# Attention with pooled queries and a two-layer network: the small scores and the ninth block at the end of a step, the row maximum in two parts

## The chip, the cores and the metric

The kernel runs on one core of a Trainium2 chip. The metric is the time of one execution on the device in microseconds (us); the time before is the median of three runs. Profiles come from one further execution, recorded by the hardware profiler.

## The reference

There are 4 batches of 8 heads, 1152 keys and a head size of 64. Two neighbouring queries are averaged, so each head has 576 queries. The output of attention, with the heads side by side, goes through two matrix products with a leaky activation between them.

```python
q_pool = q.reshape(B, H, S // 2, 2, D).mean(axis=3)
scores = scale * np.matmul(q_pool, k.transpose(0, 1, 3, 2))
scores = scores - np.max(scores, axis=-1, keepdims=True)
attn = np.exp(scores)
attn = attn / (np.sum(attn, axis=-1, keepdims=True) + 1e-09)
attn_out = np.matmul(attn, v)
x = attn_out.transpose(0, 2, 1, 3).reshape(B * S, H * D)
h = x @ w_in
g = np.maximum(h, 0.0) + alpha * np.minimum(h, 0.0)
out = g @ w_out
```

## The kernel before

**Steps.** The heads are worked in 16 pairs. The 1152 queries of a pair are nine tiles of 128; tile 4 takes 64 queries of each head. A step `s` handles one tile against all 1152 keys, so attention has 144 steps, `s % 9` is the step's place t in a round of nine, and "step 4" below means a step with t = 4. Each engine has its own instruction stream, and the order in it is written out by hand in `step` functions; engines meet by semaphores only. Odd and even steps use two buffers of scores in PSUM (`S_AT`) and two halves of `e_sb`.

**What TensorE does in step s (L575 to L604).** It waits for `exp_done`, the large exponential of tile s, and for the two slots. Then it transposes the first eight blocks of 128 columns of the tile's exponentials in 16 matmuls, one half of the 128 rows into slot 0 and the other into slot 1 (L584). It waits for `ninth_free` and for `exp_cut_done`, the small exponential of tile s + 1. Then come the small scores of tile s + 2, 128 columns (L517), the transpose of the ninth block of tile s into `NINTH` (L544), the big scores of tile s + 2, 1024 columns (L529), and a part of the product of exponentials and values (`product`, L570). `PRODUCT` says which: steps 5 to 8 work on group 0 (tiles 0 to 4 of this pair, 320 columns for each head), steps 0 to 4 on group 1 of the pair before (tiles 5 to 8, 256 columns). Nearly all take two of the nine key blocks; step 8 takes three and step 4 one. Steps 6 and 1 first spread the inverted sums of a group over the partitions (L554, into slot 0). In steps 7 and 8, `begin_scores` also waits for the keys and queries of the next pair.

**PSUM.** The small scores of both buffers and `NINTH` lie in different columns of the same bank, the third of `s_ps`. The big scores have two banks in each buffer, each slot has one, and the product has one.

**What VectorE does (L455 to L472).** It copies slot 1 to `pt` (L464) and frees the slot, copies the ninth block (L466) and frees it, and takes the negated row maximum of tile s + 2 over all 1152 columns (L431) as soon as all its scores are there (`s_ready`, 2). In steps 4 and 8 it inverts the sums of a group before that (L449, L453), in step 5 it casts x (L445). `scale` multiplies a finished product by the inverted sums (L439); it stands at the start of steps 0 and 5.

**What ScalarE does (L352 to L370).** It waits for `max_ready` of tile s + 1, takes the exponential of the 128 small columns with `accum_out` (L341), copies slot 0 to `pt` (L357), and takes the exponential of the 1024 large columns (L348). After the spreads it copies them to `inv_bc` (L363) and frees slot 0.

GpSimd sums the pairs of queries and takes the low part of x; SyncE issues the loads, of which those of values wait for `v_free`, which VectorE raises in step 5. The network behind attention is not touched, except that VectorE's first scaling there moves into the last step.

Of the kernel before, what the change touches and what calls it, by code (L numbers as in the profile page):

```python
# [7 lines left out]
ALU = mybir.AluOpType  # L8
# [3 lines left out]
P = 128  # L12
BANK = 512


def build(nc, q, k, v, w_in, w_out, alpha, out):
# [41 lines left out]
    with ExitStack() as ctx:  # L58
# [19 lines left out]
        neg_max = sb("neg_max", [P, 2])  # L78
        row_sum = sb("row_sum", [P, 2, TILES])
# [29 lines left out]
        NINTH = s_ps[:, 2 * BANK + P:2 * BANK + 2 * P]  # L109
# [20 lines left out]
        s_ready = sem("s_ready")  # L130
        max_ready = sem("max_ready")
# [3 lines left out]
        ninth_ready = sem("ninth_ready")  # L135
        slot_free = [sem(f"slot{i}_free") for i in range(2)]
        ninth_free = sem("ninth_free")
# [289 lines left out]
        def _(dve):  # L427
            def row_max(s):
                b = s % 2
                dve.wait_ge(s_ready, 2).then_inc(s_ready, -2)  # L430
                nc.vector.tensor_reduce(out=neg_max[:, b:b + 1], in_=s_ps[:, S_AT[b]:S_AT[b] + NKEY],  # L431
                                        op=ALU.max, axis=AX_X, negate=True).then_inc(max_ready, 1)
# [22 lines left out]
            def step(s, pair, left=2):  # L455
                t, g = s % TILES, s // TILES % 2
                if t == 0 and pair is not None:
                    dve.wait_ge(x_sb_free, 1).then_inc(x_sb_free, -1)
                    scale(0)
                if t == 5 and pair is not None:  # L460
                    scale(1)
                    dve.sem_inc(v_free[1 - g], 1)
                dve.wait_ge(tr_ready[1], 1).then_inc(tr_ready[1], -1)  # L463
                nc.vector.tensor_copy(pt_half(t, 1), half_columns(slot_ps[1][:, :])).then_inc(slot_free[1], 1)  # L464
                dve.wait_ge(ninth_ready, 1).then_inc(ninth_ready, -1)
                nc.vector.tensor_copy(pt_ninth(t), ninth_columns(t)).then_inc(ninth_free, 1)  # L466
# [4 lines left out]
                if left > 1:  # L471
                    row_max(s + 2)  # L472
# [20 lines left out]
            dve.sem_inc(ninth_free, 1)  # L493
            dve.sem_inc(pv_free, 1)
            row_max(0)
            row_max(1)
            over_steps(dve, step)
            dve.wait_ge(alpha_in, 16).then_inc(alpha_in, -16)
            dve.wait_ge(x_sb_free, 1).then_inc(x_sb_free, -1)
            scale(0)  # L500
# [11 lines left out]
        def _(pe):  # L512
# [62 lines left out]
            def step(s, pair, left=2):  # L575
# [12 lines left out]

                pe.wait_ge(ninth_free, 1).then_inc(ninth_free, -1)
                if left > 0:  # L590
                    pe.wait_ge(exp_cut_done, 1).then_inc(exp_cut_done, -1)  # L591
                if left > 1:
                    begin_scores(s + 2)
                    small_scores(s + 2)
                transposed(s, 2 * CH, NINTH).then_inc(ninth_ready, 1)
                if left > 1:
# [104 lines left out]
```

## Time and profile before

| | us |
|---|---|
| Median of three runs | 1018.21 (1015.3 to 1018.55) |
| The profiled execution | 1016.51 |
| Its span, first to last instruction | 1014.0 |
| Start, up to the transposes of step 8 | 58.67 |
| Steps 8 to 142 | 537.70 |
| The last step and the network | 417.63 |
| TensorE busy (matmuls) | 919.4 (91%) |
| VectorE busy | 528.3 (52%) |
| ScalarE busy | 423.4 (42%) |

Engines are called PE (TensorE matmul), PEld (TensorE weight load), DVE (VectorE), ACT (ScalarE), POOL (GpSimd) and SP (SyncE). A row of a timeline gives the start, the time that the merged instructions span, the engine and line, the output and inputs, their number, and in brackets the idle time before with what ended it. "PEq L591" is the semaphore wait in line 591. The ends of matmuls are modelled, so two groups can overlap by some hundredths; where one group follows another, the distance of the starts is the safer measure. The granted clock of TensorE is given as a share of 2.4 GHz.

### The profile page before, as it was taken

Reading aid. Unit: us, or ns where it says so; the run is one execution under the profiler, and the core shown is the slowest. Engines: PE = TensorE matmul, PEld = TensorE weight load, DVE = VectorE, ACT = ScalarE, POOL = GpSimd, SP = SyncE. Lnnn points to the kernel's source line nnn. Section 1 sums busy time; section 2 is a strip of 40 time slices with the busy share of each in tenths; the row PEclk is TensorE's granted clock in tenths of the full one; section 3 lists DMA queues with packets and bytes.
Section 4 is the critical chain, followed back from the end, with each engine's and each line's share of the span. In section 5 each row is a group of like instructions: output and inputs, shape, how many; then the busy total and the mean of one; then the engine's idle time right before and its main releaser. Section 6 shows DMA issues by size and latency. Waiting matters only on the chain. (4 is left out here: it accounts for less than half of the span.)

```text
span 1014.0 us, 20768 instructions
## 1 busy us (share of the span) xinstructions
PE 919.4 (91%) x6896; PEld 632.5 (62%) x6896; DVE 528.3 (52%) x836; ACT 423.4 (42%) x963; POOL 213.6 (21%) x182
## 2 busy tenths in 40 slices
PE   3798888889889888888888889999999999999997
PEld 1344444444444444444444459999999999999996
DVE  1456666666666666666666644444444444444442
ACT  1455555555555555555555542222232222322222
POOL 2011112102111111211111023333333333333331
PEclk9899999999999999999999999999999999999999
DMA  7334134224423413532442012122232222422211
GB/s 171 97 77 123 49 75 122 64 57 122 104 63 76 122 47 75 122 87 60 96 121 65 1 32 63 62 62 63 62 125 62 62 63 62 126 63 67 60 48 62
DMA packets 36366, 79.57 MB, mean 78 GB/s; under 512 B 5360, under 2 KB 9456, under 8 KB 36336
## 3 DMA queue, kind: packets, MB, share of 16 engines
q1 hardware_dynamic: 33936, 74.48, 28.4%
q10 hardware_dynamic: 2400, 4.72, 1.3%
q8 instruction: 16, 0.26, 0.1%
q14 instruction: 14, 0.11, 0.0%
HBM read 74.46 MB, written 4.72 MB: 78 GB/s over the span
## 5 line engine op out<-in xcount | busy, mean ns | idle before, releaser
L431 DVE TENSOR_REDUCE neg_max<-s_ps 128x1 f32<-128x1152 f32 x144 | 195.5, 1357 | 111.3 <-DVEq L430 111.3
L529 PE MATMUL s_ps<-k_f,q_f 64*128 64x512 f32 (+1 forms) x640 | 167.6, 657 | 5.2 <-PEq L540 5.2
L570 PE MATMUL pv_ps<-pt,v_f 128*64 128x256 f32 (+1 forms) x1152 | 170.3, 417 | 0.0
L348 ACT ACTIVATE e_sb<-s_ps,neg_max 128x1024 f32<-128x1024 f32 x144 | 160.3, 1113 | 0.0
L341 ACT ACTIVATE e_sb<-s_ps,neg_max 128x128 f32<-128x128 f32 x144 | 53.0, 368 | 221.2 <-ACTq L340 221.1
L570 PEld LDWEIGHTS pv_ps<-pt,v_f 128*64 128x64 f32 x1152 | 71.4, 137 | 112.5 <-issue 82.8
L464 DVE COPY pt<-slot_ps 128x512 f32<-128x512 f32 x144 | 99.5, 691 | 75.6 <-DVEq L463 75.5
L517 PE MATMUL s_ps<-k_end,q_f 128*128 128x128 f32 (+1 forms) x320 | 68.1, 317 | 77.6 <-PEq L591 56.4
L584 PEld LDWEIGHTS slot_ps<-ident,e_sb 64*128 64x128 f32 x2304 | 86.1, 141 | 71.1 <-issue 71.1
L613 PE MATMUL slot_ps<-x_hi,wi_hi 128*128 128x384 f32 x384 | 129.5, 337 | 1.0 <-PEq L609 1.0
L613 PE MATMUL slot_ps<-x_lo,wi_hi 128*128 128x384 f32 x384 | 129.5, 337 | 0.0
L613 PE MATMUL slot_ps<-x_hi,wi_lo 128*128 128x384 f32 x384 | 129.0, 336 | 0.0
L477 DVE TENSOR_SCALAR e_sb<-slot_ps,alpha_sb 128x384 f32<-128x384 f32 x96 | 59.3, 618 | 123.7 <-DVEq L475 123.7
L584 PE MATMUL slot_ps<-ident,e_sb 64*128 64x64 f32 x2304 | 104.6, 231 | 4.0 <-PEq L579 3.8
L486 DVE TENSOR_TENSOR g_lo<-e_sb,g_hi 128x384 fp32r<-128x384 f32 x96 | 53.6, 559 | 99.2 <-DVEq L485 99.2
L517 PEld LDWEIGHTS s_ps<-k_end,q_f 128*128 128x128 f32 (+1 forms) x320 | 42.6, 182 | 93.4 <-issue 91.4
L628 PE MATMUL s_ps<-wo_lo,g_hi 128*128 128x512 f32 x240 | 95.1, 396 | 0.0
L628 PE MATMUL s_ps<-wo_hi,g_lo 128*128 128x512 f32 x240 | 94.8, 395 | 0.0
L628 PE MATMUL s_ps<-wo_hi,g_hi 128*128 128x512 f32 x240 | 93.3, 389 | 1.1 <-PEq L625 1.1
L272 POOL TENSOR_TENSOR q_raw<-q_raw 128x576 f32<-128x576 f32 x32 | 44.9, 1404 | 234.4 <-POOLq L271 234.4
L357 ACT ACTIVATE pt<-slot_ps 128x512 f32<-128x512 f32 x144 | 85.1, 591 | 19.5 <-ACTq L356 19.5
L303 POOL TENSOR_TENSOR wo_lo<-wo_raw,wo_hi 128x512 fp32r<-128x512 f32 x48 | 62.0, 1292 | 139.1 <-POOLq L302 139.1
(46 smaller groups left out, 1006.3 us busy)
## 6 DMA issues: line engine op xcount, KB each, us to landing
q_raw<-in_q SPq DMA_DIRECT2D x64, 288.0 KB, 4.6
k_f<-in_k SPq DMA_DIRECT2D x64, 288.0 KB, 4.1
wi_raw<-in_w_in SPq DMA_DIRECT2D x48, 256.0 KB, 2.6
wo_raw<-in_w_out SPq DMA_DIRECT2D x48, 256.0 KB, 2.6
v_f<-in_v SPq DMA_DIRECT2D x32, 288.0 KB, 3.1
out<-pt ACTq DMA_DIRECT2D x6, 768.0 KB, 4.6
k_end<-in_k SPq DMA_DIRECT2D x64, 32.0 KB, 4.0
alpha_sb<-in_alpha SPq DMA_DIRECT2D x1, 8.0 KB, 4.7
```

Of the source, the lines that this page charges most:

```text
L303: nc.gpsimd.tensor_tensor(wo_lo[i][:, :], wo_raw[i][:, :], wo_hi[i][:, :].bitcast(F32), ALU.subtract).then_inc(pool_self, 1)
L348: nc.scalar.activation(e_sb[:, b * NKEY + at:b * NKEY + at + n], s_ps[:, S_AT[b] + at:S_AT[b] + at + n], ACT.Exp, bias=neg_max[:, b:b + 1] ...
L357: nc.scalar.activation(pt_half(t, 0), half_columns(slot_ps[0][:, :]), ACT.Copy).then_inc(slot_free[0], 1)
L431: nc.vector.tensor_reduce(out=neg_max[:, b:b + 1], in_=s_ps[:, S_AT[b]:S_AT[b] + NKEY], op=ALU.max, axis=AX_X, negate=True).then_inc(max_r ...
L464: nc.vector.tensor_copy(pt_half(t, 1), half_columns(slot_ps[1][:, :])).then_inc(slot_free[1], 1)
L477: nc.vector.tensor_scalar(neg_sb, hid, 0.0, alpha_sb[:, bass.ds(f, 1)], ALU.min, ALU.mult).then_inc(dve_self, 1)
L517: ins = nc.tensor.matmul(s_ps[to:to + m, S_AT[b] + at:S_AT[b] + at + P], q_f[2 * g + h][:, first:first + m], k_end[2 * g + h][:, end, :], ...
L529: ins = nc.tensor.matmul(s_ps[to:to + m, S_AT[b] + at:S_AT[b] + at + BANK], q_f[2 * g + h][rows, first:first + m], k_f[2 * g + h][rows, at ...
L570: ins = nc.tensor.matmul(pv_ps[h * D:(h + 1) * D, 0:n], v_f[2 * g + h][:, a, :], pt[:, a, at:at + n], start=(a == 0), stop=(a == KT - 1))
L584: ins = nc.tensor.transpose(slot_ps[i][:, a * HALF:(a + 1) * HALF], e_sb[rows, at:at + P], ident[rows, rows])
L613: ins = nc.tensor.matmul(slot_ps[h][:, 0:TOK], w[i][:, d * P:(d + 1) * P], x[:, at:at + TOK], start=(d == 0 and w is wi_hi and x is x_hi), ...
L628: ins = nc.tensor.matmul(y_ps[h][t], g[h][:, t * P:(t + 1) * P], w[i][:, :], start=(first == 0 and j == 0), stop=(last == 1 and j == 2))
```

## The change

In TensorE's step, the big scores of tile s + 2 follow the transposes of tile s directly, then comes the product, and at the step's end the transpose of the ninth block, the wait for `exp_cut_done`, and the small scores of tile s + 2. `NINTH` now lies in the first 128 columns of slot 1; so the slot is taken and freed twice in a step, and `ninth_free` is gone. VectorE takes the maximum over the 1024 large columns (`big_max`) once the big scores are there, and the maximum over the 128 small columns with the minimum of the two negated values (`row_max`) at the start of the next step. The scalings move from the start of steps 0 and 5 to steps 8 and 4, ahead of the copy of the ninth block, which is now last in VectorE's step.

```diff
-        NINTH = s_ps[:, 2 * BANK + P:2 * BANK + 2 * P]
+        NINTH = slot_ps[1][:, 0:P]
...
-            def row_max(s):
+            def big_max(s):
                 b = s % 2
                 dve.wait_ge(s_ready, 2).then_inc(s_ready, -2)
-                nc.vector.tensor_reduce(out=neg_max[:, b:b + 1], in_=s_ps[:, S_AT[b]:S_AT[b] + NKEY],
-                                        op=ALU.max, axis=AX_X, negate=True).then_inc(max_ready, 1)
+                nc.vector.tensor_reduce(out=neg_big[:, b:b + 1],
+                                        in_=s_ps[:, S_AT[b] + BIG_AT[b]:S_AT[b] + BIG_AT[b] + 2 * BANK],
+                                        op=ALU.max, axis=AX_X, negate=True).then_inc(max_self, 1)
+            def row_max(s):
+                b = s % 2
+                dve.wait_ge(s_end_ready, 1).then_inc(s_end_ready, -1)
+                nc.vector.tensor_reduce(out=neg_end[:, b:b + 1],
+                                        in_=s_ps[:, S_AT[b] + END[b][0]:S_AT[b] + END[b][0] + P],
+                                        op=ALU.max, axis=AX_X, negate=True).then_inc(max_self, 1)
+                dve.wait_ge(max_self, 2).then_inc(max_self, -2)
+                nc.vector.tensor_tensor(neg_max[:, b:b + 1], neg_big[:, b:b + 1], neg_end[:, b:b + 1],
+                                        ALU.min).then_inc(max_ready, 1)
...
             def step(s, pair, left=2):
                 t, g = s % TILES, s // TILES % 2
-                if t == 0 and pair is not None:
-                    dve.wait_ge(x_sb_free, 1).then_inc(x_sb_free, -1)
-                    scale(0)
-                if t == 5 and pair is not None:
-                    scale(1)
-                    dve.sem_inc(v_free[1 - g], 1)
+                if left > 0:
+                    row_max(s + 1)
                 dve.wait_ge(tr_ready[1], 1).then_inc(tr_ready[1], -1)
                 nc.vector.tensor_copy(pt_half(t, 1), half_columns(slot_ps[1][:, :])).then_inc(slot_free[1], 1)
-                dve.wait_ge(ninth_ready, 1).then_inc(ninth_ready, -1)
-                nc.vector.tensor_copy(pt_ninth(t), ninth_columns(t)).then_inc(ninth_free, 1)
+                if left > 1:
+                    big_max(s + 2)
                 if t in INVERT:
                     invert(INVERT[t])
                 if t == 5 and pair is not None:
                     x_high(pair + (0 if s < 2 * TILES else 1))
-                if left > 1:
-                    row_max(s + 2)
+                if t == 4 and s >= TILES:
+                    scale(1)
+                    dve.sem_inc(v_free[1 - g], 1)
+                if t == 8:
+                    dve.wait_ge(x_sb_free, 1).then_inc(x_sb_free, -1)
+                    scale(0)
+                dve.wait_ge(ninth_ready, 1).then_inc(ninth_ready, -1)
+                nc.vector.tensor_copy(pt_ninth(t), ninth_columns(t)).then_inc(slot_free[1], 1)
...
-                pe.wait_ge(ninth_free, 1).then_inc(ninth_free, -1)
-                if left > 0:
-                    pe.wait_ge(exp_cut_done, 1).then_inc(exp_cut_done, -1)
                 if left > 1:
                     begin_scores(s + 2)
-                    small_scores(s + 2)
-                transposed(s, 2 * CH, NINTH).then_inc(ninth_ready, 1)
-                if left > 1:
                     for ins in big_scores(s + 2):
                         ins.then_inc(s_ready, 1)
                 group, tiles = PRODUCT[t]
...
                     product(group, g if group == 0 else 1 - g, tiles)
+                pe.wait_ge(slot_free[1], 1).then_inc(slot_free[1], -1)
+                transposed(s, 2 * CH, NINTH).then_inc(ninth_ready, 1)
+                if left > 0:
+                    pe.wait_ge(exp_cut_done, 1).then_inc(exp_cut_done, -1)
+                if left > 1:
+                    small_scores(s + 2).then_inc(s_end_ready, 1)
```

## Rows read from the trace of the kernel before

**Rows 1.** Stretches: the steady part of attention, steps 8 to 142.

```profile
core 0: us, PE busy (x) PEld busy (x) DVE busy (x) ACT busy (x) POOL busy (x), PEclk, DMA share, GB/s
58.67:596.37 537.70, 473.45 (x4572) 246.23 (x4571) 337.50 (x510) 293.05 (x705) 77.16 (x69) 1.00 0.33 81
```

**Rows 2.** The page's groups: busy us, mean ns, idle before, releaser.

```profile
L431 DVE TENSOR_REDUCE neg_max<-s_ps 128x1 f32<-128x1152 f32 x144 | 195.5, 1357 | 111.3 <-DVEq L430 111.3
L517 PE MATMUL s_ps<-k_end,q_f 128*128 128x128 f32 (+1 forms) x320 | 68.1, 317 | 77.6 <-PEq L591 56.4
```

**Rows 3.** Timeline of TensorE: start us, us; steps 6, 8, 0, 3, 4, 5.

```profile
412.07 0.77 PE L554 MATMUL slot_ps<-ident,inv_sum 128*64 128x128 f32 x12
412.67 1.25 PE L570 MATMUL pv_ps<-pt,v_f 128*64 128x320 f32 x8
413.91 0.71 PE L584 MATMUL slot_ps<-ident,e_sb 64*128 64x64 f32 x16
...
420.56 1.83 PE L570 MATMUL pv_ps<-pt,v_f 128*64 128x320 f32 x12
422.32 0.71 PE L584 MATMUL slot_ps<-ident,e_sb 64*128 64x64 f32 x16
422.96 0.49 PE L517 MATMUL s_ps<-k_end,q_f 128*128 128x128 f32 x2
...
436.34 1.08 PE L570 MATMUL pv_ps<-pt,v_f 128*64 128x256 f32 x8
437.35 0.71 PE L584 MATMUL slot_ps<-ident,e_sb 64*128 64x64 f32 x16
...
438.97 0.27 PE L544 MATMUL s_ps<-ident,e_sb 128*128 128x128 f32 x1
439.17 1.13 PE L529 MATMUL s_ps<-k_f,q_f 64*128 64x512 f32 x4
440.23 0.65 PE L570 MATMUL pv_ps<-pt,v_f 128*64 128x256 f32 x4
440.82 0.71 PE L584 MATMUL slot_ps<-ident,e_sb 64*128 64x64 f32 x16
442.57 0.46 PE L517 MATMUL s_ps<-k_end,q_f 128*128 128x128 f32 x2 [1.04 <-PEq L591]
...
443.07 1.13 PE L529 MATMUL s_ps<-k_f,q_f 64*128 64x512 f32 x4
```

**Rows 4.** Timeline of VectorE: the scalings, step 4, and step 5.

```profile
422.58 0.49 DVE L439 TENSOR_TENSOR x_sb<-pv_ps,inv_bc 128x320 f32<-128x320 f32 x1 [0.41 <-DVEq L438]
423.42 0.69 DVE L464 COPY pt<-slot_ps 128x512 f32<-128x512 f32 x1 [0.35 <-DVEq L463]
...
439.39 0.29 DVE L466 COPY pt<-s_ps 128x128 f32<-128x128 f32 x1 [0.45 <-DVEq L465]
439.60 0.16 DVE L449 SCALAR_TENSOR_TENSOR sum_eps<-row_sum 128x5 f32<-128x5 f32 x1
439.90 0.19 DVE L453 RECIPROCAL inv_sum<-sum_eps 128x5 f32<-128x5 f32 x1
440.49 1.36 DVE L431 TENSOR_REDUCE neg_max<-s_ps 128x1 f32<-128x1152 f32 x1 [0.39 <-DVEq L430]
441.76 0.41 DVE L439 TENSOR_TENSOR x_sb<-pv_ps,inv_bc 128x256 f32<-128x256 f32 x1
442.62 0.69 DVE L464 COPY pt<-slot_ps 128x512 f32<-128x512 f32 x1 [0.44 <-DVEq L463]
...
443.50 0.45 DVE L445 CAST x_hi<-x_sb 128x576 f32 x1
```

**Rows 5.** Timeline of ScalarE: the exponentials in step 5.

```profile
441.97 0.37 ACT L341 ACTIVATE e_sb<-s_ps,neg_max 128x128 f32<-128x128 f32 x1 [1.85 <-ACTq L340]
442.23 0.19 ACT L341 ACTIVATION_READ_ACCUMULATOR e_sb<-s_ps,neg_max 128x1 f32 x1
...
443.80 0.21 ACT L348 ACTIVATION_READ_ACCUMULATOR e_sb<-s_ps,neg_max 128x1 f32 x1
```

**Rows 6.** Stretches: two pieces of the first round, columns as in rows 1.

```profile
39.00:41.00 2.00, 1.04 (x18) 0.61 (x16) 1.49 (x2) 0.15 (x3) 0.00 (x0) 1.00 0.00 0
45.00:47.00 2.00, 1.52 (x5) 1.11 (x7) 0.80 (x2) 1.92 (x5) 0.00 (x0) 0.50 0.00 0
```

More of the change, by code:

```diff
@@ L78, in build @@
         neg_max = sb("neg_max", [P, 2])
+        neg_big = sb("neg_big", [P, 2])
+        neg_end = sb("neg_end", [P, 2])
         row_sum = sb("row_sum", [P, 2, TILES])
@@ L130, in build @@
         s_ready = sem("s_ready")
+        max_self = sem("max_self")
         max_ready = sem("max_ready")
@@ L135, in build @@
         ninth_ready = sem("ninth_ready")
+        s_end_ready = sem("s_end_ready")
         slot_free = [sem(f"slot{i}_free") for i in range(2)]
-        ninth_free = sem("ninth_free")
         inv_ready = sem("inv_ready")
@@ L427, in _ @@
         def _(dve):
+            def big_max(s):
+                b = s % 2
+                dve.wait_ge(s_ready, 2).then_inc(s_ready, -2)
+                nc.vector.tensor_reduce(out=neg_big[:, b:b + 1],
+                                        in_=s_ps[:, S_AT[b] + BIG_AT[b]:S_AT[b] + BIG_AT[b] + 2 * BANK],
+                                        op=ALU.max, axis=AX_X, negate=True).then_inc(max_self, 1)
             def row_max(s):
                 b = s % 2
-                dve.wait_ge(s_ready, 2).then_inc(s_ready, -2)
-                nc.vector.tensor_reduce(out=neg_max[:, b:b + 1], in_=s_ps[:, S_AT[b]:S_AT[b] + NKEY],
-                                        op=ALU.max, axis=AX_X, negate=True).then_inc(max_ready, 1)
+                dve.wait_ge(s_end_ready, 1).then_inc(s_end_ready, -1)
[5 more added lines that the diff above has]
+                                        ALU.min).then_inc(max_ready, 1)
             def scale(group):
@@ L492, in _ @@
                 dve.sem_inc(slot_free[i], 1)
-            dve.sem_inc(ninth_free, 1)
             dve.sem_inc(pv_free, 1)
+            big_max(0)
             row_max(0)
-            row_max(1)
+            big_max(1)
             over_steps(dve, step)
             dve.wait_ge(alpha_in, 16).then_inc(alpha_in, -16)
-            dve.wait_ge(x_sb_free, 1).then_inc(x_sb_free, -1)
-            scale(0)
             for n in range(PASSES):
@@ L637, in _ @@
             begin_scores(0)
-            small_scores(0)
+            small_scores(0).then_inc(s_end_ready, 1)
             for ins in big_scores(0):
@@ L641, in _ @@
             begin_scores(1)
-            big_scores(1)
+            for ins in big_scores(1):
+                ins.then_inc(s_ready, 1)
             pe.wait_ge(exp_cut_done, 1).then_inc(exp_cut_done, -1)
-            small_scores(1).then_inc(s_ready, 2)
+            small_scores(1).then_inc(s_end_ready, 1)
             over_steps(pe, step)
@@ L650, in _ @@
             pe.wait_ge(slot_free[1], 1)
-            pe.wait_ge(ninth_free, 1).then_inc(ninth_free, -1)
             product(1, 1, (0, 1))
```

## The prediction

> **What bounds the kernel now.** I first asked the stretches of the profile where the time lies. The steady part of attention runs from the transposes of step 8 to those of step 143, 135 steps, 537.70 us, or 35.85 us for each round of nine steps [rows 1]. The change touches only this part and the eight steps ahead of it, so nothing is expected to move in the feed-forward part. TensorE is busy in 473 of these 537.70 us. That share alone would suggest an engine near its limit, but the groups of instructions on the page show a hole: before the small scores TensorE stood idle for 77.6 us, 56.4 of it at L591, the wait for `exp_cut_done` [rows 2].
>
> Next I followed one hole through the timelines of three engines. The big scores of step 4 start at 439.17 [rows 3]. The row maximum starts at 440.49, 1.32 later, and takes 1.36, to 441.85 [rows 4]. The cut exponential starts 0.12 later, at 441.97, and its accumulator read ends at 442.42 [rows 5]. TensorE's small scores start 0.15 later, at 442.57, after 1.04 of idle time, and the next big scores at 443.07 [rows 3]. The loop is closed: 1.32 + 1.36 + 0.12 + 0.45 + 0.15 + 0.50 = 3.90 us for a step. Nine such steps are 35.1; the round has 0.75 more, since steps with a spread (0.60), with the third product tile or with new keys are longer on TensorE alone. So the kernel is bound by a ring through three engines, with the row maximum as its longest piece. TensorE has slack in most steps, and VectorE's other work (inversion, scaling, the cast of x) lies in VectorE's own holes, beside the ring.
>
> **What the change does to that ring.** The big scores no longer stand behind `exp_cut_done`. They follow the transposes at once. From transposes to the next matmul it takes 0.64 when nothing is late (422.32 to 422.96), from big scores to product 1.06 (439.17 to 440.23) [rows 3]. A product of two tiles takes 1.01 for 256 columns (436.34 to 437.35) and 1.24 for 320 (412.67 to 413.91), one tile 0.59 (440.23 to 440.82), three tiles 1.76 (420.56 to 422.32), all from start to the next group's start [rows 3]. The wait at L591 goes away: `exp_cut_done` is now asked for only at the step's end.
>
> **What it adds.** The reduction of 1152 columns is split. Copies of 512 and of 128 columns took 0.69 and 0.29 [rows 4], which is 1.04 ns for each column more; a reduction of 1024 columns is then, as an estimate, 1.36 - 128 x 1.04 ns = 1.23, and one of 128 about 0.29. The minimum of two columns has no row; the nearest is the 128x5 operation with 0.15 to 0.16, then 0.14 until the dependent one starts [rows 4]. Its bounds are 0.1 and 0.3. The end maximum, the minimum and their gap, 0.6 together, stand at the start of the next step while TensorE transposes (0.71), and VectorE could copy the half only when that is done. So I cost them at nothing there. If that cover went they would cost 0.6 in each step.
>
> The small maximum is also the head of the exponentials' chain: with the small scores ending about when the next transposes start, the minimum is out 0.64 after that start, the cut exponential starts at 0.76, and from the cut's start to the end of the large exponential's accumulator read are 2.04 (441.97 to 444.01) [rows 5], then 0.15 to TensorE: 2.95. Every step below is longer, so this chain waits for nobody.
>
> The ninth block is the piece that matters. Before, its copy was released to TensorE most of a step ahead of its use, as it had its own columns. Now it is put into slot 1, and the next step's transposes wait for `slot_free[1]`. If N is the start of the ninth transpose, its copy starts at N + 0.42 (438.97 to 439.39) and takes 0.29 [rows 3, 4]. From the copy's end to a matmul on TensorE there is no row; ScalarE to TensorE took 0.15, VectorE to ScalarE 0.12 [rows 3, 5]. I take 0.15. So the transposes start at N + 0.86, where TensorE alone, with 0.20 for the ninth block and 0.30 for the small scores out of the 0.50 above, would be ready at N + 0.50. This is a new wait of 0.36.
>
> And VectorE must reach that copy: in its queue stand, ahead of it, the large maximum, in steps 4 and 8 the inversion and a scaling, in step 5 the cast. The large maximum starts 0.64 + 1.32 = 1.96 after the transposes and ends at 3.19. A following instruction that is not late starts 0.08 before that end (439.60 against 439.39 + 0.29), so at 3.11. A scaling takes 0.84 to 0.86 until the next copy starts (422.58 to 423.42, 441.76 to 442.62), the inversion 0.30 and 0.19 [rows 4].
>
> **The sum, step by step**, each from its transposes to the next ones. Steps 0, 2 and 3: N = 0.64 + 1.06 + 1.01 = 2.71, copy at 3.13, next step at 3.57. Step 1: a spread of eight matmuls, 0.5 (between two thirds of the 0.60 that twelve took and all of it), gives 4.07. Step 4: inversion from 3.11 to 3.60, scaling from 3.52, copy at 4.38, next step at 4.82. Step 5: the cast (0.45) from 3.11, copy at 3.48, next step at 3.92. Step 6: 0.64 + 1.06 + 0.60 + 1.24 + 0.86 = 4.40. Step 7: 3.80. Step 8: the product starts at 1.70 and its last matmul ends 1.83 later, the scaling starts 0.19 after that end (422.58 against 422.39) at 3.72, copy at 4.56, next step at 5.00. The sum is 36.72 a round against 35.85: the bare steps win 0.33 each, and steps 4 and 8 give back more than all of it, because the scaling now stands between TensorE and its slot. Over 15 rounds that is +13.0. In the first eight steps there is no scaling, and about four bare steps win 0.33: -1.4. In all +11.6 us. The profiled execution took 1016.5 us (its span is 1014.0), the median is 1018.2; I set the forecast against the median: about 1029.
>
> The Trainium skill (VectorE: DVE Perf Modes, "Rules for kernel authors") advises to minimise the number of VectorE operations, which speaks against two instructions more in each step. By that rule alone, VectorE's time grows by about 0.32 a step, 46 us over 144 steps if VectorE were the bound; by the rows, it stood idle for 111.3 us before the row maxima alone [rows 2], and the sum charges nothing for the split itself.
>
> **Rivals.**
> *The hand-back is cheap (the other side).* If VectorE hands a slot to TensorE in less than 0.15, all nine steps shorten, as all end on that hand-over. The point from which it decides is 11.6 / 135 = 0.09 us less than taken, that is 0.06. At zero the sum is 11.6 - 20.3 = -8.7, 1009.5 us. Against it: both cross-engine hand-overs in the rows took 0.12 to 0.15. For it: no row shows this pair.
> *No change.* The gaps of 0.35 and 0.44 behind a scaling [rows 4] might not be paid in steps 4 and 8. Then a round is 0.8 shorter, the total -12, and the time 1018. Against it: the copy behind the scaling at 441.76 had its data already (those transposes, from 440.82, were over at 441.53) [rows 3, 4], so the gap belongs to the semaphore instructions behind the scaling, and these stay.
> *The clock falls.* In the first round, where a step had no product of the other group, TensorE was busy for 1.04 of 2.00 us, and shortly after ran at 0.50 of its clock, the 1.2 GHz level [rows 6]. Step 4 would now be busy for 2.8 of 4.82 us, with some 2.0 idle in one piece. If the clock fell there in every round, step 5's matmuls, 3.44 us at the full level, would need 6.9, which is 3.0 above the 3.92 of the sum: +45 us, 1074; in half of the rounds, 1051. Against it: before, step 5 bore 1.04 of idle time in one piece [rows 3] at a clock of 1.00 in the whole stretch [rows 1]. The Trainium skill (TensorE: Matmul & The Clock Gate, "What's actually happening") says that the throttled state is the default and activity releases it; by it this case is possible in a step so empty, and the trace agrees in the first round.
> *Waits laid bare.* Between the short small scores and the transposes TensorE now handles three waits. The gap of 0.44 behind a scaling had four semaphore instructions [rows 4], about 0.1 each. If 0.1 a step came on top it would be +13.5, 1043.
>
> **How the numbers follow.** The forecast as summed, with or without some bare waits, has 0.55; the clock 0.13; the cheap hand-back 0.18; no change 0.12; the rest is for what I have not seen. A difference of 0.3% is about what a measurement of this kernel tells from no change. The steps of the sum are built from rows that repeat to a hundredth, but an error of 0.1 in the common hand-over alone moves the total by 13.5, so the range goes from near the cheap hand-back, 1010, to half the clock case, 1051. Faster 0.18, same 0.13, slower 0.69.
>
> **What would show it.** Right: idle time before the transposes with the wait for the slot as releaser, some 0.36 in steps 1, 6 and 7 and over 1 in steps 4 and 8; no idle time before the big scores; bare steps of 3.57; a large maximum of 1.23; the minimum out before the half's copy. Wrong: bare steps near 3.4 would mean a cheap hand-back, matmuls of the big scores with twice their time the clock case, and a late large exponential before the transposes a chain that I take for hidden.

## The result, and the profile after

The changed kernel took 1049.1 us (median; 1046.19 to 1050.17), the kernel before 1017.7. The ratio is 1.0308, with a 95% interval of 1.0279 to 1.0337: slower, as forecast, but by 31 us where 11 were forecast, and inside the range (1010 to 1051) only by a hair. The profiled execution took 1050.17 us, with a span of 1047.3.

The page of the changed kernel, busy time by engine and three of its groups (busy us, mean ns, idle before and its releaser):

```profile
PE 910.0 (87%) x6896; PEld 631.0 (60%) x6896; DVE 584.1 (56%) x1124; ACT 418.5 (40%) x963; POOL 213.3 (20%) x182
...
L435 DVE TENSOR_REDUCE neg_big<-s_ps 128x1 f32<-128x1024 f32 x144 | 176.1, 1223 | 53.4 <-DVEq L434 52.9
L600 PE MATMUL slot_ps<-ident,e_sb 64*128 64x64 f32 x2304 | 105.2, 231 | 90.7 <-PEq L595 90.7
...
L545 PE MATMUL s_ps<-k_f,q_f 64*128 64x512 f32 (+1 forms) x640 | 168.5, 647 | 5.3 <-PEq L556 5.3
```

The wait for `exp_cut_done`, 56.4 us before [rows 2], is gone, and the big scores no longer wait for it. In its place stand 90.7 us of idle time ahead of the transposes, ended by L595, the wait for the slots. The large maximum takes 1223 ns, as estimated.

The stretches, with the granted clock behind the five busy times:

```profile
50.39:629.62 579.23, 471.41 (x4570) 248.02 (x4571) 390.30 (x779) 288.43 (x705) 77.10 (x69) 0.97 0.31 75
629.62:1047.00 417.38, 409.80 (x2089) 368.41 (x2089) 169.13 (x295) 110.53 (x212) 125.19 (x97) 1.00 0.23 70
0.00:50.39 50.39, 28.83 (x238) 14.57 (x239) 24.63 (x51) 19.59 (x46) 11.06 (x16) 1.00 0.59 141
```

The same cuts as before: up to the transposes of step 8 it took 50.39 us against 58.67, from there to the transposes of step 143 it took 579.23 against 537.70 [rows 1], and the rest is unchanged. So the first eight steps won 8.3 us and the 15 rounds lost 41.5. The granted clock in the rounds was 0.97, where it had been 1.00 [rows 1].

Now one hole, in steps 4 and 5 of a round. The timeline of TensorE, VectorE and the first ScalarE operation:

```profile
419.32 0.72 PE L600 MATMUL slot_ps<-ident,e_sb 64*128 64x64 f32 x16 [0.36 <-PEq L595]
...
419.84 1.11 PE L545 MATMUL s_ps<-k_f,q_f 64*128 64x512 f32 x4
...
421.10 1.22 DVE L435 TENSOR_REDUCE neg_big<-s_ps 128x1 f32<-128x1024 f32 x1 [0.23 <-DVEq L434]
421.46 0.33 PE L560 MATMUL slot_ps<-ident,e_sb 128*128 128x128 f32 x1
421.63 0.39 PE L533 MATMUL s_ps<-k_end,q_f 128*128 128x128 f32 x2
...
422.24 0.15 DVE L465 SCALAR_TENSOR_TENSOR sum_eps<-row_sum 128x5 f32<-128x5 f32 x1
422.54 0.19 DVE L469 RECIPROCAL inv_sum<-sum_eps 128x5 f32<-128x5 f32 x1
422.80 0.42 DVE L455 TENSOR_TENSOR x_sb<-pv_ps,inv_bc 128x256 f32<-128x256 f32 x1
423.67 0.29 DVE L490 COPY pt<-slot_ps 128x128 f32<-128x128 f32 x1 [0.44 <-DVEq L489]
...
424.11 0.71 PE L600 MATMUL slot_ps<-ident,e_sb 64*128 64x64 f32 x16 [2.09 <-PEq L595]
424.30 0.16 DVE L447 TENSOR_TENSOR neg_max<-neg_big,neg_end 128x1 f32<-128x1 f32 x1
424.58 0.37 ACT L344 ACTIVATE e_sb<-s_ps,neg_max 128x128 f32<-128x128 f32 x1 [2.68 <-ACTq L343]
```

The step is 4.79 us long (4.82 forecast). TensorE starts its last work at 421.63 and then stands idle for 2.09 us, while VectorE works through maximum, inversion, scaling and the copy of the ninth block. That copy ends at 423.96 and the transposes start at 424.11: the hand-over from VectorE to TensorE, for which no row stood before, takes 0.15. In the rounds of this trace it takes 0.15 at the end of every step but one, so it is this hand-back of slot 1, and not a late exponential, that lets the transposes start.

Two things are in the trace that the forecast did not have. One is the clock. These are stretches around the end of another step 4 and the step 5 behind it, the last a part of the one before it:

```profile
148.00:152.00 4.00, 1.90 (x27) 1.20 (x26) 2.72 (x8) 1.27 (x4) 0.00 (x0) 1.00 0.05 6
152.00:156.00 4.00, 4.00 (x19) 1.47 (x15) 2.28 (x3) 1.91 (x5) 0.74 (x1) 0.58 0.91 274
...
153.00:155.00 2.00, 2.00 (x10) 0.77 (x8) 1.59 (x2) 0.91 (x2) 0.00 (x0) 0.50 0.95 292
```

TensorE was busy in 1.90 of 4.00 us and then ran at 0.50, its lower level of 1.2 GHz. And here is a step 1, with the small maximum and the minimum on VectorE, GpSimd, the small exponential and the copy of slot 0 on ScalarE, and the spread on TensorE:

```profile
95.75 0.29 DVE L443 TENSOR_REDUCE neg_end<-s_ps 128x1 f32<-128x128 f32 x1
96.03 1.40 POOL L275 TENSOR_TENSOR q_raw<-q_raw 128x576 f32<-128x576 f32 x1 [8.26 <-POOLq L274]
96.19 1.26 DVE L447 TENSOR_TENSOR neg_max<-neg_big,neg_end 128x1 f32<-128x1 f32 x1
97.37 0.68 DVE L476 COPY pt<-slot_ps 128x512 f32<-128x512 f32 x1
97.57 0.37 ACT L344 ACTIVATE e_sb<-s_ps,neg_max 128x128 f32<-128x128 f32 x1 [2.58 <-ACTq L343]
...
97.93 0.59 ACT L360 ACTIVATE pt<-slot_ps 128x512 f32<-128x512 f32 x1
...
98.81 0.66 PE L570 MATMUL slot_ps<-ident,inv_sum 128*64 128x128 f32 x8 [1.22 <-PEq L565]
```

The minimum of one element in each partition takes 1.26 us instead of 0.16, and it ends 0.02 after GpSimd's sum of queries does (97.43). In the whole trace 23 of the 144 minima took 0.45 to 1.29 us. All 23 started while one of GpSimd's operations at L275 or L290 was running, both of which read two operands in SBUF, and ended 0.01 to 0.02 after it. One more minimum overlapped such an operation, but had started 0.10 ahead of it, and took its usual 0.16.

What the delay costs is in the last three rows. ScalarE copies slot 0 behind the small exponential, which waits for the minimum, and in steps 1 and 6 the spread needs slot 0. TensorE stands idle for 1.22 us ahead of it. (The row names L565, the last of two waits that stand there; the inverse that L565 waits for was ready a step earlier, so the wait is the one for slot 0.) In the two steps 1 whose minimum was not held, this idle time is 0.12.

The length of each kind of step, from its transposes to the next ones, worked out from the starts in the timeline as the mean over the 14 or 15 rounds:

| step | before | forecast | after | after, shortest |
|---|---|---|---|---|
| 0 | 3.24 | 3.57 | 3.49 | 3.48 |
| 1 | 4.56 | 4.07 | 4.91 | 4.11 |
| 2 | 3.32 | 3.57 | 3.60 | 3.59 |
| 3 | 3.91 | 3.57 | 3.49 | 3.48 |
| 4 | 3.46 | 4.82 | 4.79 | 4.78 |
| 5 | 4.54 | 3.92 | 4.80 | 3.72 |
| 6 | 4.52 | 4.40 | 5.01 | 4.42 |
| 7 | 3.56 | 3.80 | 3.66 | 3.70 (usual) |
| 8 | 4.73 | 5.00 | 4.87 | 4.87 |

(The ring of 3.90 in the kernel before runs from big scores to big scores; counted so, each kind of step took 3.87 to 4.24 there.) Where steps are undisturbed they are within 0.2 of the forecast, mostly within 0.1. Steps 1, 5 and 6 are not undisturbed. Their means are above their shortest by 0.80, 1.08 and 0.59, together 2.47 a round or 37 us. That is more than the whole loss of 31, and it set the questions for the experiments.

### The profile page after: what moved, and what is told of

It reads as the page before. It is cut to its first block and busy times, and to the rows that moved or that the text cites. A ratio compares the mean times of both kernels' runs of the same rounds, so it can differ in the third digit from the quotient of the medians.

```text
span 1047.3 us, 21342 instructions
## 1 busy us (share of the span) xinstructions
PE 910.0 (87%) x6896; PEld 631.0 (60%) x6896; DVE 584.1 (56%) x1124; ACT 418.5 (40%) x963; POOL 213.3 (20%) x182
## 5 line engine op out<-in xcount | busy, mean ns | idle before, releaser
L435 DVE TENSOR_REDUCE neg_big<-s_ps 128x1 f32<-128x1024 f32 x144 | 176.1, 1223 | 53.4 <-DVEq L434 52.9
L600 PE MATMUL slot_ps<-ident,e_sb 64*128 64x64 f32 x2304 | 105.2, 231 | 90.7 <-PEq L595 90.7
L586 PE MATMUL pv_ps<-pt,v_f 128*64 128x256 f32 (+1 forms) x1152 | 176.8, 428 | 0.0
L600 PEld LDWEIGHTS slot_ps<-ident,e_sb 64*128 64x128 f32 x2304 | 89.2, 141 | 114.9 <-issue 114.9
L586 PEld LDWEIGHTS pv_ps<-pt,v_f 128*64 128x64 f32 x1152 | 75.8, 140 | 117.3 <-issue 90.9
L476 DVE COPY pt<-slot_ps 128x512 f32<-128x512 f32 x144 | 99.3, 690 | 58.7 <-DVEq L475 58.4
L275 POOL TENSOR_TENSOR q_raw<-q_raw 128x576 f32<-128x576 f32 x32 | 45.0, 1406 | 227.2 <-POOLq L274 227.2
L298 POOL TENSOR_TENSOR wi_lo<-wi_raw,wi_hi 128x512 fp32r<-128x512 f32 x48 | 61.8, 1287 | 137.0 <-POOLq L297 137.0
L290 POOL TENSOR_TENSOR x_lo<-x_sb,x_hi 128x576 f32 (+1 forms) x16 | 22.4, 1403 | 305.4 <-POOLq L289 305.4
```

The source lines that it names most:

```text
L298: nc.gpsimd.tensor_tensor(wi_lo[i][:, :], wi_raw[i][:, :], wi_hi[i][:, :].bitcast(F32), ALU.subtract).then_inc(pool_self, 1)
L435: nc.vector.tensor_reduce(out=neg_big[:, b:b + 1], in_=s_ps[:, S_AT[b] + BIG_AT[b]:S_AT[b] + BIG_AT[b] + 2 * BANK], op=ALU.max, axis=AX_X, ...
L586: ins = nc.tensor.matmul(pv_ps[h * D:(h + 1) * D, 0:n], v_f[2 * g + h][:, a, :], pt[:, a, at:at + n], start=(a == 0), stop=(a == KT - 1))
L600: ins = nc.tensor.transpose(slot_ps[i][:, a * HALF:(a + 1) * HALF], e_sb[rows, at:at + P], ident[rows, rows])
```

## The experiments

All ratios are against the kernel before, run on the same chip in alternation. The first three experiments take the two disturbances apart; the order is that of the argument.

**The small maximum in PSUM.** The minimum then has one operand in PSUM.

```diff
-        neg_end = sb("neg_end", [P, 2])
+        neg_end = s_ps[:, NKEY:NKEY + 2]
```

> The small maximum is written to two free columns of PSUM instead of SBUF, so the minimum reads one operand from PSUM; nothing else changes. Theory A (the minimum is held up when GpSimd runs an operation on two SBUF operands, because both want the same way into SBUF): the 23 long minima (0.45 to 1.29 us) all become about 0.16, step 1 falls from a mean of 4.91 to 4.11 and the blocked part of steps 6 goes, together 12 to 20 us: 1029 to 1037. Rival B (the long minima only mark something else, such as a late small maximum, or any VectorE operation is held by GpSimd): the long operations stay, 1049.

Measured: 1034.2 us, 1.0176 (1.0154 to 1.0198), 15 us less than the changed kernel. The minima's line, first of the changed kernel, then of this one (ns, shortest, median and longest):

```profile
L447 DVE TENSOR_TENSOR neg_max<-neg_big,neg_end x144: 158/159/1294, 13.5 to 626.9; 128x1 f32<-128x1 f32 x144
```

```profile
L447 DVE TENSOR_TENSOR neg_max<-neg_big,s_ps x144: 154/154/157, 13.5 to 608.5; 128x1 f32<-128x1 f32 x144
```

No minimum took more than 157 ns, though GpSimd's operations of 1.4 us overlapped 26 of them. Step 1 had 4.12 in every round and step 6 fell to 4.59. Rival B is out, and theory A holds as far as it says which operand matters; that it is a shared way into SBUF no run shows by itself. Step 5 kept its 4.82, so it has another cause.

**The hole of step 4 filled.** Three matmuls on keys that are in place anyway, into slot 0; their result is not used.

```diff
+                if t == 4 and pair is not None:
+                    pe.wait_ge(slot_free[0], 1)
+                    for _ in range(3):
+                        nc.tensor.matmul(slot_ps[0][:, :], ident[:, :], k_f[2 * g][:, 0:BANK], start=True, stop=True)
```

> The changed kernel with three more matmuls of 128x512 at the end of step 4, whose result nobody reads, so that TensorE is busy in what was its hole of 2.1 us. Theory C (step 5 is long in most rounds because the clock falls to 1.2 GHz behind that hole): with the hole filled the clock stays at 1.00, step 5 falls from a mean of 4.80 to 3.72, and the time falls by about 16 us, to 1033, though TensorE does more work. Rival D (the long steps 5 come from VectorE or a late pv_free): step 5 stays at about 5.25 in ten rounds of fifteen and the time at 1049 or above.

Measured: 1047.0 us, 1.0293 (1.0271 to 1.0316). The time was missed, the mechanism was not. Stretches of the rounds, first the changed kernel, then this one:

```profile
50.00:628.00 578.00, 470.61 (x4567) 247.87 (x4568) 390.22 (x779) 287.26 (x704) 77.30 (x70) 0.97 0.31 75
```

```profile
50.00:628.00 578.00, 494.70 (x4674) 257.79 (x4672) 395.64 (x781) 289.90 (x706) 77.90 (x71) 1.00 0.31 76
```

The clock is at 1.00 and step 5 had 3.75 to 3.83 in all rounds but the first (4.07, with no loss of clock there before either). So the long steps 5 are the clock's. The gain was eaten twice. The three matmuls were too many, as these lines of a step 4 show:

```profile
382.62 2.74 PE L624 MATMUL slot_ps<-k_f,ident 128*128 128x512 f32 x6
...
384.44 0.29 DVE L490 COPY pt<-slot_ps 128x128 f32<-128x128 f32 x1 [0.44 <-DVEq L489]
...
385.29 0.72 PE L600 MATMUL slot_ps<-ident,e_sb 64*128 64x64 f32 x16
```

The copy had ended at 384.73, and the transposes came at 385.29: step 4 went to 5.20. And with rounds that are now all alike, nearly every one met GpSimd in steps 1 and 6: 29 long minima with 24.8 us over 0.16 each, against 23 with 18.3 in the changed kernel. When a disturbance is a meeting of two engines in time, curing another one can make it more frequent.

**Both cures.** The small maximum in PSUM, and two matmuls in the hole, not three.

```diff
-        neg_end = sb("neg_end", [P, 2])
+        neg_end = s_ps[:, NKEY:NKEY + 2]
...
+                    for _ in range(2):
```

> Both cures of the excess at once and nothing else: the changed kernel with the small maximum in PSUM and two (not three) matmuls of 128x512 in the hole of step 4, whose result nobody reads. If the clock and the held-up minimum are the whole of what the forecast missed, every step takes its undisturbed length (3.49, 4.12, 3.60, 3.49, 4.79, 3.72, 4.42, 3.70, 4.87), 36.2 a round, and the time is 1049 less 15 x 2.4 = 36, that is 1012 to 1014. If a third cause is in it, the time stays above 1020.

Measured: 1016.2 us, 0.9995 (0.9985 to 1.0006). The stretch of the rounds:

```profile
49.99:595.56 545.57, 481.69 (x4629) 251.72 (x4630) 375.56 (x779) 288.16 (x705) 77.16 (x69) 1.00 0.33 80
```

A round takes 36.4 us, and the loss of 31 us is gone. It is 2 us over the expected time, as step 6 took 4.58 instead of 4.42 on average. It alternates: some 4.80 in one round and 4.42 in the next. The trace shows what goes with it. The steps are written as a loop over two rounds, whose body begins with a step 6, so in every second round all engines jump back just ahead of it. Here is VectorE at a step 6 that begins the body, and at the next step 6, inside the body:

```profile
187.10 0.28 DVE L490 COPY pt<-slot_ps 128x128 f32<-128x128 f32 x1
187.67 0.30 DVE L443 TENSOR_REDUCE s_ps<-s_ps 128x1 f32<-128x128 f32 x1 [0.28 <-DVEq L442]
```

```profile
223.98 0.29 DVE L443 TENSOR_REDUCE s_ps<-s_ps 128x1 f32<-128x128 f32 x1
```

At the jump the trace has a comparison and branch of VectorE between the starts of the two rows, and the small maximum starts 0.14 behind the step's transposes (187.53), where at 223.98 it starts 0.23 ahead of them. The spread then waits for slot 0 for 0.48 instead of 0.10. The six steps 6 that a jump back leads into are the six long ones (4.79 to 4.86; the step 5 ahead of them is 0.1 shorter). No run moves the jump, so this is read from the trace alone. There is no other cause of the size of the two disturbances. The re-ordering by itself, without the clock and the held minimum, comes out level: 7.9 us more in the rounds, 8.7 less in the first eight steps.

**How GpSimd holds the minimum.** The same two operands in SBUF, but only one of them as a tensor:

```diff
-                nc.vector.tensor_tensor(neg_max[:, b:b + 1], neg_big[:, b:b + 1], neg_end[:, b:b + 1],
-                                        ALU.min).then_inc(max_ready, 1)
+                nc.vector.tensor_scalar(neg_max[:, b:b + 1], neg_big[:, b:b + 1], neg_end[:, b:b + 1], 1.0,
+                                        ALU.min, ALU.mult).then_inc(max_ready, 1)
```

> The changed kernel, with the minimum written as a tensor_scalar operation: neg_big as its only tensor operand and neg_end as a per-partition scalar, both in SBUF. If what GpSimd holds up is a VectorE operation with two tensor operands in SBUF, no minimum takes longer than 0.2 us and the time is that of the run with the small maximum in PSUM, 1034. If any minimum whose operands are in SBUF is held up, about 20 long ones stay and the time is 1049.

Measured: 1034.6 us, 1.0165 (1.0132 to 1.0199), the time of the run with PSUM. The minima's line:

```profile
L447 DVE TENSOR_SCALAR neg_max<-neg_big,neg_end x144: 212/214/217, 13.7 to 610.9; 128x1 f32<-128x1 f32 x144
```

30 of these minima overlapped a GpSimd operation. What matters is that both operands are read as tensors from SBUF: with one of them in PSUM, or read as one scalar for each partition, the minimum isn't held.

This run shows one thing more. Its minimum is 0.06 longer than that of the run with PSUM, and it costs some 0.05 in each step 1 (4.17 against 4.12) and in the shortest step 6 (4.47 against 4.42), and nothing in the steps without a spread. So in steps 1 and 6 the chain from the small maximum over the minimum to slot 0 has no slack at all, even where nothing is held.

**The cost of the split alone.** The kernel before, with both parts of the maximum behind one another:

```diff
-                nc.vector.tensor_reduce(out=neg_max[:, b:b + 1], in_=s_ps[:, S_AT[b]:S_AT[b] + NKEY],
-                                        op=ALU.max, axis=AX_X, negate=True).then_inc(max_ready, 1)
+                nc.vector.tensor_reduce(out=neg_big[:, b:b + 1],
+                                        in_=s_ps[:, S_AT[b] + BIG_AT[b]:S_AT[b] + BIG_AT[b] + 2 * BANK],
+                                        op=ALU.max, axis=AX_X, negate=True).then_inc(max_self, 1)
+                nc.vector.tensor_reduce(out=neg_end[:, b:b + 1],
+                                        in_=s_ps[:, S_AT[b] + END[b][0]:S_AT[b] + END[b][0] + P],
+                                        op=ALU.max, axis=AX_X, negate=True).then_inc(max_self, 1)
+                dve.wait_ge(max_self, 2).then_inc(max_self, -2)
+                nc.vector.tensor_tensor(neg_max[:, b:b + 1], neg_big[:, b:b + 1], neg_end[:, b:b + 1],
+                                        ALU.min).then_inc(max_ready, 1)
```

> The kernel before with only the row maximum in two parts, one behind the other once all scores are there, and the minimum. It has the cost of the split without the early start. The ring of 3.90 us grows by 1.23 + 0.29 + 0.14 + 0.16 - 0.08 - 1.36 = 0.38 in each of about 140 steps: 50 us, 1068, and a little more if GpSimd holds up some minima. Rival (the row maximum is not in the ring): 1017.

Measured: 1068.9 us, 1.0509 (1.0481 to 1.0537). The ring in its timeline:

```profile
434.39 1.13 PE L539 MATMUL s_ps<-k_f,q_f 64*128 64x512 f32 x4
...
435.70 1.22 DVE L434 TENSOR_REDUCE neg_big<-s_ps 128x1 f32<-128x1024 f32 x1 [0.80 <-DVEq L433]
...
436.84 0.28 DVE L437 TENSOR_REDUCE neg_end<-s_ps 128x1 f32<-128x128 f32 x1
437.27 0.16 DVE L441 TENSOR_TENSOR neg_max<-neg_big,neg_end 128x1 f32<-128x1 f32 x1
...
437.55 0.37 ACT L344 ACTIVATE e_sb<-s_ps,neg_max 128x128 f32<-128x128 f32 x1 [2.22 <-ACTq L343]
...
438.65 1.13 PE L539 MATMUL s_ps<-k_f,q_f 64*128 64x512 f32 x4
```

From big scores to big scores it is 4.26 us, against 3.90 in [rows 3]. The reading of the kernel before as a ring with the row maximum in it is confirmed by a forecast that met the time to 1 us. In the changed kernel the same split costs next to nothing in the steps without a spread, where the hand-back of slot 1 ends later.

**The scalings in the next step.** In the changed kernel, `scale(1)` and `scale(0)` go back to steps 5 and 0, there behind `row_max(s + 1)`.

```diff
                 if left > 0:
                     row_max(s + 1)
+                if t == 0 and pair is not None:
+                    dve.wait_ge(x_sb_free, 1).then_inc(x_sb_free, -1)
+                    scale(0)
+                if t == 5 and pair is not None:
+                    scale(1)
+                    dve.sem_inc(v_free[1 - g], 1)
...
-                if t == 4 and s >= TILES:
-                    scale(1)
-                    dve.sem_inc(v_free[1 - g], 1)
-                if t == 8:
-                    dve.wait_ge(x_sb_free, 1).then_inc(x_sb_free, -1)
-                    scale(0)
```

> Only the place of the two scalings is put back to the next step (steps 5 and 0), there behind the small maximum and the minimum and ahead of the copy of the half. If the scalings ahead of the ninth copy are what makes steps 4 and 8 long: step 4 from 4.79 to 3.9, step 8 from 4.87 to 4.2, steps 5 and 0 at most 0.25 longer, and as the hole in step 4 shrinks from 2.1 to about 1.2 the clock stays up, which gives 1.08 a round more: in all 1.1 + 1.1 = 2.2 a round, 33 us, 1016. If the clock falls all the same, only half of that, 1033. Rival (the place of the scalings costs nothing, the wait is elsewhere): 1049.

Measured: 1008.5 us, 0.9914 (0.9891 to 0.9937): faster than the kernel before. Step 4 took 3.81, step 8 4.24, step 5 3.87 and step 0 3.60. The clock of the whole run was 0.998. In the rounds the clock was at 1.00, behind a hole in step 4 of 1.11 us where the changed kernel has 2.09. It beat the expected 1016 because step 1 now met GpSimd once in 15 rounds instead of 13 times (4.17 on average instead of 4.91, 11 us); step 6 met it in all 15 (5.39 instead of 5.01), which took half of that back. With the small maximum in PSUM as well:

> The scalings in the next step (as in the run with 1008.5) and the small maximum in PSUM. The 16 long minima there held 14.3 us; if each cost its step what it took too long, the time falls by 13 to 15 us to about 994. If the chain behind them has slack, by less than 8, to above 1000.

Measured: 994.1 us, 0.9784 (0.9764 to 0.9804). 14.4 us less for 14.3 us of held minima (in the rounds alone 13.9): as in the run with `tensor_scalar`, the chain has hardly any slack in these steps.

**The ninth block in the middle.** Transposed between big scores and product, its copy ahead of the large maximum; scalings as in the changed kernel.

```diff
                     for ins in big_scores(s + 2):
                         ins.then_inc(s_ready, 1)
+                pe.wait_ge(slot_free[1], 1).then_inc(slot_free[1], -1)
+                transposed(s, 2 * CH, NINTH).then_inc(ninth_ready, 1)
                 group, tiles = PRODUCT[t]
...
-                pe.wait_ge(slot_free[1], 1).then_inc(slot_free[1], -1)
-                transposed(s, 2 * CH, NINTH).then_inc(ninth_ready, 1)
```

> The ninth block is transposed between the big scores and the product, and its copy stands ahead of the large maximum; the small scores stay at the end of the step. Then slot 1 is free before the step ends. Theory (the hand-back of slot 1 at the step's end binds every step): the idle time before the transposes of 90.7 us almost vanishes; bare steps go from 3.49 to 3.2 or 3.3, step 4 from 4.79 to about 3.4, step 8 from 4.87 to 4.1, and the clock stays up: 33 to 34 us a round against 38.6, 70 us less, about 980. Rival (the chain over maximum, minimum and exponentials takes over at once, as the large maximum now ends later): bare steps stay at 3.5, about 1000 to 1010.

Measured: 1026.9 us, 1.0108 (1.0084 to 1.0133), slower than both expectations. Its group of the transposes:

```profile
L600 PE MATMUL slot_ps<-ident,e_sb 64*128 64x64 f32 x2304 | 103.2, 229 | 14.6 <-PEq L595 13.8
```

The wait for the slots fell from 90.7 to 13.8 us, as expected, step 3 fell from 3.49 to 3.37 and step 2 from 3.60 to 3.42. But steps 5 and 0 took 4.88 and 4.08. The scaling of step 8 now runs into the next step, and the lines of that step show what is queued behind it:

```profile
461.80 0.71 PE L600 MATMUL slot_ps<-ident,e_sb 64*128 64x64 f32 x16
461.84 0.49 DVE L455 TENSOR_TENSOR x_sb<-pv_ps,inv_bc 128x320 f32<-128x320 f32 x1 [0.19 <-DVEq L454]
...
463.27 0.69 DVE L476 COPY pt<-slot_ps 128x512 f32<-128x512 f32 x1
...
464.10 0.30 PE L560 MATMUL slot_ps<-ident,e_sb 128*128 128x128 f32 x1 [0.68 <-PEq L608]
```

The half's copy is late, the ninth block waits for the slot that it frees, and the product stands behind the ninth block. Also, 26 minima were held, by 28.3 us in all. Neither expectation named this; the part of it on the clock was right (0.998). With the small maximum in PSUM:

> The ninth block between big scores and product, and the small maximum in PSUM, scalings as in the changed kernel. 26 long minima held 28.3 us in the run without the move to PSUM. Held-up minimum: step 1 to 3.9, step 6 to 4.3, about 27 us less, 1000. Steps 5 and 0 stay at 4.9 and 4.1, because the scaling stands ahead of the small maximum, or, if step 5 is the clock, it stays between 3.9 and 4.9.

Measured: 999.7 us, 0.9834 (0.9814 to 0.9854). Step 5 stayed at 4.89 with a clock of 0.999, so it is the queue and not the clock. With the scalings in the next step too:

> All three: the ninth block in the middle, the scalings behind the next step's minimum, the small maximum in PSUM. If nothing but TensorE and the chain over the exponentials is left as bound: bare steps 3.4, step 1 3.9, step 4 3.4, step 5 3.6, step 6 4.2, step 7 3.6, step 8 4.15, 33.1 a round, 41 us under the kernel before: about 970 to 975. If VectorE's queue is the next bound (scaling and inversion push the large maximum), 34.5 a round and 992.

Measured: 1005.7 us, 0.9895 (0.9876 to 0.9915), 6 us slower than without the last move, and a clear miss. Step 0 went to 4.38 and step 5 stayed at 4.91: put ahead of the half's copy on purpose, the scaling delays the same slot as before. Both moves are good, but each undoes the cover of the other.

**A mixture.** The ninth block in the middle, except in steps 0 and 5, with scalings in the next step and the small maximum in PSUM.

```diff
+                if t not in (0, 5):
+                    pe.wait_ge(slot_free[1], 1).then_inc(slot_free[1], -1)
+                    transposed(s, 2 * CH, NINTH).then_inc(ninth_ready, 1)
                 group, tiles = PRODUCT[t]
...
-                pe.wait_ge(slot_free[1], 1).then_inc(slot_free[1], -1)
-                transposed(s, 2 * CH, NINTH).then_inc(ninth_ready, 1)
+                if t in (0, 5):
+                    pe.wait_ge(slot_free[1], 1).then_inc(slot_free[1], -1)
+                    transposed(s, 2 * CH, NINTH).then_inc(ninth_ready, 1)
                 if left > 0:
                     pe.wait_ge(exp_cut_done, 1).then_inc(exp_cut_done, -1)
```

> Built from the lengths measured so far: the ninth block in the middle of the step, but at the end in steps 0 and 5, where the scalings stand ahead of the half's copy; small maximum in PSUM. If step lengths carry over one by one: 3.61, 3.93, 3.43, 3.37, 3.43, 3.87, 4.38, 3.60, 4.15 for steps 0 to 8, 33.8 a round, 977. If steps are coupled (a step that is freed of its wait hands it on to the next), 34.6 a round or more, 989 or more.

Measured: 991.7 us, 0.9756 (0.9734 to 0.9777), the fastest of all, but 15 us over the sum of step lengths. Steps 0 and 5 took 4.04 and 4.63, not 3.61 and 3.87. A step's length is not its own: step 4 is now so short that VectorE enters step 5 late, with its inversion still to do:

```profile
454.64 0.71 PE L606 MATMUL slot_ps<-ident,e_sb 64*128 64x64 f32 x16 [0.42 <-PEq L601]
454.70 0.16 DVE L465 SCALAR_TENSOR_TENSOR sum_eps<-row_sum 128x5 f32<-128x5 f32 x1
...
455.15 0.30 DVE L443 TENSOR_REDUCE s_ps<-s_ps 128x1 f32<-128x128 f32 x1
...
456.73 1.30 PE L592 MATMUL pv_ps<-pt,v_f 128*64 128x320 f32 x8 [0.47 <-PEq L589]
```

The product then waits for the scaling to free its bank (L589). Scalings behind the half's copy, where they would stand ahead of neither hand-back of slot 1, were not tried with the ninth block in the middle.

## Why the prediction was wrong in size

**What held.** The ring before, the vanished wait at L591, the estimate of 1.23 for the large maximum (1223 ns), the hand-over of 0.15, and the new wait for slot 1 of 0.36 (0.36 at the end of steps 3 and 7 too, 419.32 in the rows above) were as worked out. So was the mechanism behind the direction: steps 4 and 8 give back what the bare steps win, because scaling and inversion stand between TensorE and its slot. Moving only the scalings out of that place turned the loss into a gain, 1049.1 to 1008.5. The sum of the steps was 36.72 forecast and 36.37 measured with both disturbances out, 5 us less over 15 rounds. Part of that: I took 0.64 from transposes to big scores; it was 0.52 (419.32 to 419.84), since no wait stands between them any more.

**The step that failed first** is "the end maximum, the minimum and their gap, 0.6 together, stand at the start of the next step while TensorE transposes ... So I cost them at nothing there", and, of the exponentials' chain, "so this chain waits for nobody". Both looked only at the half's copy and at the next step's transposes. In steps 1 and 6 something nearer waits on that chain, the spread, which needs slot 0 from ScalarE behind the small exponential. There the cover was nothing even for a minimum of 0.16, as the run with `tensor_scalar` shows; it went unseen because the undisturbed wait is only 0.12 and 0.10 us. In these steps the minimum took up to 1.29, held behind GpSimd, and TensorE waited for slot 0 by the same amount more, 1.22 in the rows shown. The cause is shown twice, by an operand in PSUM and by a scalar operand; it costs 15 us by the medians (18 in the rounds of the traces, for 18.3 us of held minima). The jump of the loop comes into the same chain, for another 2 us. The sum had no term and the rivals had no case for it, although both were to be had: GpSimd's 1.40 us operations are in the profile before, and the Trainium skill (SBUF — State Buffer, "SBUF: two separate sides") says that a VectorE operation with two SBUF inputs and a GpSimd operation that reads SBUF take an exclusive lock on a shared pair of ports. The trace agrees: 1.26 against 0.16, ending with GpSimd's operation. The forecast costed the minimum by its size alone, between 0.1 and 0.3. GpSimd's sums in the kernel before:

```profile
L272 POOL TENSOR_TENSOR q_raw<-q_raw 128x576 f32<-128x576 f32 x32 | 44.9, 1404 | 234.4 <-POOLq L271 234.4
```

**The second** is the weight of a rival that was named. "If the clock fell there in every round ... +45 us ... Against it: before, step 5 bore 1.04 of idle time in one piece" got 0.13. Step 4's hole was 2.09 us, as forecast ("some 2.0 idle in one piece"), and the clock fell behind it in ten of 15 rounds. The price was over-estimated: a long step 5 took some 5.3, not 6.9, for the clock was back before its end (its mean over the ten long steps 5 was 0.67 to 0.70); the mean excess was 1.08 a round, 16 us. A hole of 1.04 that the clock survives says nothing of one that is twice as long. Filling the hole restored the clock to 1.00, and so did shortening it to 1.11 us with the scalings in the next step, which shows the cause. The Trainium skill (TensorE: Matmul & The Clock Gate, "What's actually happening") has activity release the throttled state; here, too, the trace agrees.

The two together are 33 us, from 1049.1 to 1016.2 with both cured. With neither, the forecast of 1029 would have been 13 us too high: 5 from steps that are a little shorter than summed, and 7 from the third miss. So the range held by luck: its upper end of 1051 was the clock in half of the rounds alone, and what filled it was the clock at a lower price and the held minimum together.

**The third** is the first eight steps, -1.4 forecast and -8.3 measured. There the changed kernel left the lower clock earlier. (The first stretch of the profile after gives a PEclk of 1.00 all the same; the lengths of equal matmuls show the level.) In its timeline four matmuls of big scores take 1.11 us from 24.95 on, where in the kernel before they take 2.08 at 28.05; first after, then before:

```profile
24.95 1.11 PE L545 MATMUL s_ps<-k_f,q_f 64*128 64x512 f32 x4
```

```profile
28.05 2.08 PE L529 MATMUL s_ps<-k_f,q_f 64*128 64x512 f32 x4
```

It also did not fall back as the kernel before did [rows 6]. Whether that follows from the order or from where the start happened to fall, no experiment was made to tell; but in each of the eleven kernels run with the changed kernel's order or one derived from it the big scores of tile 3 were at the full level, at 23.8 to 25.3 us, and in the two with the old order, the kernel before and the split alone, they still took twice the time, at 28.1 and 28.9. The eleven reached step 8 at 48.8 to 52.1 us (the three that fell back once on the way at 51.1 to 52.1), the two at 58.7 and 61.6. So the order is the likelier reason, from one trace of each kernel; it is argued and not shown.

What stays open: why the same hole of 2.1 us is followed by the lower clock in ten rounds and not in the other five, and what in the new order lifts the clock earlier at the start.

## What to carry to other kernels

A short operation that a change adds to a chain should be costed by what else uses its ports while it runs, not by its size: a minimum of one element took 1.29 us behind another engine's operation, and giving it one PSUM or one scalar operand made that vanish. Before work is called covered, ask of every engine that waits for what follows it, and not only of the next one: here the cover held for the copy and the transposes, and not for the spread. When a change trades many short waits of TensorE for few long ones, check the clock behind the longest, because a hole of 2.09 us was followed by the lower clock in ten of 15 rounds, and holes of 1.04 and 1.11 in none of the rounds. And where engines hand a buffer round each step, put side work (scalings, inversions) behind the hand-over and not ahead of it, then time the step after it too, since steps do not add.

## What was not expected of the hardware

- GpSimd operations of 1.40 us on two SBUF operands held a one-element VectorE `tensor_tensor` on two SBUF operands for up to 1.29 us. In the changed kernel all 23 that started during such an operation were held, and the one that had started ahead of it was not. The same operation with one operand in PSUM (at most 157 ns) or with one as a per-partition scalar (at most 217 ns) was never held in 144 executions each, of which 26 and 30 overlapped one of GpSimd's. A reduction of 128 PSUM columns kept its 0.29 us while GpSimd's operation ran (427.95 in the trace after, with GpSimd from 427.77).
- The jump of a loop body is not free on a chain without slack: VectorE's first operation behind it started 0.37 us later in its step than without it (187.67 against 223.98 above), and the step took 0.37 us more.
- The same idle hole of 2.1 us in step 4 led to the lower clock in ten rounds of 15 and to none in the other five. One round read alone can miss it.
